# Moving the sum of tap products to TensorE, and reordering ScalarE and TensorE around the first turning, in a fused mix and two-FFN kernel

## The reference

```python
# per token s and head h: seven taps over the tokens s-6 .. s
w = softmax(weight_gen)                      # over the last axis, 7 taps
x = sum over k of w[s, h, k] * x_pad[s + k]  # 8 heads of 24 columns, D = 192
# gated FFN, 1536 wide
xn = x / sqrt(mean(x*x) + 1e-6) * rms_g
x = (silu(xn @ w_gate) * (xn @ w_val)) @ w_out
# second FFN, 2048 wide
h = x @ w_in
out = (h * (1 / (1 + exp(-1.702 * h)))) @ w_out2
```

## Time and profile before

| | us |
|---|---|
| median of 3 runs | 1227.09 |
| lowest, highest | 1226.65, 1227.09 |
| the profiled execution | 1227.05 |
| its span in the trace | 1225.1 |

### The profile page before, as it was taken

How to read it: one execution, slowest core, us unless ns; L and a number is a source line. 1 busy time by engine, 2 the same in 40 slices (tenths; PEclk the granted TensorE clock), 3 DMA queues, 4 the chain that set the end, 5 groups by cost and what they waited for, 6 DMA issues and landing times.

```text
span 1225.1 us, 28909 instructions
## 1 busy us (share of the span) xinstructions
PE 1214.6 (99%) x12025; PEld 1047.0 (85%) x12025; DVE 794.9 (65%) x1245; ACT 662.0 (54%) x1180; POOL 59.5 (5%) x65
## 2 busy tenths in 40 slices
PE   8999999999999999999999999999999999999998
PEld 5989999888898888988888888888988889888888
DVE  7887584855839567494774848658385674944533
ACT  5655555455554555646455454555645556454554
POOL 4323000000000000000000000000000000000000
PEclk9999999999999999999999999999999999999999
DMA  7220010100101001010010001000010010000000
GB/s 206 85 67 32 18 33 2 50 2 18 33 5 47 1 19 33 18 34 2 18 34 18 33 2 37 15 18 34 5 47 1 18 34 2 14 1 14 1 15 14
DMA packets 15457, 33.10 MB, mean 27 GB/s; under 512 B 1892, under 2 KB 8804, under 8 KB 15328
## 3 DMA queue, kind: packets, MB, share of 16 engines
q1 hardware_dynamic: 15328, 31.26, 8.0%
HBM read 24.96 MB, written 6.29 MB: 26 GB/s over the span
## 4 chain that ended last, share of the span: by engine, by line
PE 96%; DVE 1%; DMA 1%; ACT 1%; issue 0%; SPq 0%; POOL 0%; ACTq 0%; DVEq 0%
PE up_ps L996 52%; PE acc L996 40%; PE up_ps L1000 2%; PE acc L1000 2%; DMA x_win<-in_x_dram 0%; DMA stage<-in_moe_w_val_dram 0%; DVE h_lo L953 0%; PE acc L1260 0%; PE acc L1268 0%; DVE hidden L942 0%; ACT o_lo L610 0%; ACT h_hi L652 0%; ACT L628 0%; POOL rms_stat L502 0%; ACT hidden L645 0%
## 5 line engine op out<-in xcount | busy, mean ns | idle before, releaser
L953 DVE TENSOR_TENSOR h_lo<-hidden,h_hi 128x512 fp32r<-128x512 f32 x448 | 314.3, 702 | 320.9 <-ACT h_hi L652 320.4
L652 ACT CAST h_hi<-hidden 128x512 fp32r<-128x512 f32 x448 | 278.1, 621 | 244.9 <-DVE hidden L942 234.0
L996 PE MATMUL acc<-out_w,h_hi 64*128 64x384 f32 x1024 | 300.3, 354 | 0.0
L1000 PE MATMUL acc<-out_w,h_hi 64*128 64x384 f32 x1024 | 299.7, 353 | 0.0
L645 ACT ACTIVATE hidden<-up_ps 128x512 f32<-128x512 f32 x256 | 152.5, 596 | 193.8 <-PE up_ps L1000 193.6
L996 PE MATMUL acc<-out_w,h_lo 64*128 64x192 f32 x1024 | 253.1, 247 | 0.0
L1000 PE MATMUL acc<-out_w,h_lo 64*128 64x192 f32 x1024 | 253.0, 247 | 0.0
L996 PE MATMUL up_ps<-x_hi,up_w 64*128 64x512 f32 x752 | 236.7, 394 | 0.0
L1000 PE MATMUL up_ps<-x_hi,up_w 64*128 64x512 f32 x752 | 234.8, 392 | 0.0
L996 PE MATMUL acc<-h_hi,out_w 64*128 64x512 f32 x576 | 195.5, 393 | 2.4 <-DVE y_f L889 1.3
L996 PEld LDWEIGHTS acc<-out_w,h_lo 64*128 64x128 f32 x1024 | 191.3, 187 | 5.2
(11 more groups left out here) (145 smaller groups left out, 3202.8 us busy)
## 6 DMA issues: line engine op xcount, KB each, us to landing
x_win<-in_x_dram SPq DMA_DIRECT2D x14, 960.0 KB
out_dram<-out_sb SPq DMA_DIRECT2D x15, 384.0 KB, 2.3
stage<-in_moe_w_out_dram SPq DMA_DIRECT2D x13, 192.0 KB, 3.5
logits<-in_weight_gen_dram SPq DMA_DIRECT2D x16, 112.0 KB, 2.0
stage<-in_moe_w_in_dram SPq DMA_DIRECT2D x4, 256.0 KB, 2.9
stage<-in_moe_w_gate_dram SPq DMA_DIRECT2D x3, 256.0 KB, 5.0
stage<-in_moe_w_gate_dram SPq DMA_DIRECT2D x5, 128.0 KB, 4.9
stage<-in_moe_w_val_dram SPq DMA_DIRECT2D x5, 128.0 KB, 5.1
```

What stands on the lines that cost most here:

```text
L652: nc.scalar.copy(h_hi[:, u % 4, :], hidden[:, u % 2, :]).then_inc(hi_ready, 1)
L953: nc.vector.tensor_tensor(h_lo[:, u % 4, :], hidden[:, u % 2, :], h_hi[:, u % 4, :].bitcast(F32), ALU.subtract).then_inc(lo_ready, 1)
L996: return nc.tensor.matmul(ps, w[TOP], data[TOP], start=start, stop=stop)
L1000: return nc.tensor.matmul(ps, w[LOW], data[LOW], start=start, stop=stop)
```

## The change

TAPS_PE goes from 4 to 6: the first six products go to buffers of their own and TensorE adds them (two matmuls for each product, each recorded as two instructions); the seventh goes to `mixed`, and VectorE's two additions of products among themselves are gone. On ScalarE the squares of x(0) stand behind the first rounded copy and ahead of the second and third; copy_left(1) goes from ahead of copy 4 to behind round_main(0); the small Silu that loads its table, and copy 4, go behind copy_twin(0). Copies 6 and 7 go from ahead of block 0 into it (HI_FIRST 8 to 6). On TensorE leave(0) is followed by eight rehearsals, then leave(1), the turning and leave(2); the other rehearsals behind the taps are gone.

```diff
-    TAPS_PE = 4
+    TAPS_PE = TAPS - 1
...
-    HI_FIRST = 8
+    HI_FIRST = HI_POOL + 1
...
+        first_taps += [tap[:, 0, :, :], tap[:, 1, :, :]]
...
             mix_exp(0)
-            for n in range(3):
-                chunk_hi_half(n)
+            chunk_hi_half(0)
+            mix_square(0)
+            chunk_hi_half(1)
+            chunk_hi_half(2)
             copy_left(0)
-            mix_square(0)
             chunk_hi_half(3)
-            copy_left(1)
-            chunk_hi_half(4)
             mix_exp(1)
             act.wait_ge(g_ready, 2)
             round_main(0)
-            nc.scalar.activation(warm[:, :], g_main[:, :], ACT.Silu)
+            copy_left(1)
             copy_left(2)
             copy_twin(0)
-            for n in range(HI_POOL + 1, HI_FIRST):
-                chunk_hi_half(n)
+            nc.scalar.activation(warm[:, :], g_main[:, :], ACT.Silu)
+            chunk_hi_half(4)
             all_blocks(run)
...
-                    to = first_taps[k] if k < TAPS_PE else (mixed, tap[:, 0, :, :], tap[:, 1, :, :])[k - TAPS_PE]
+                    to = first_taps[k] if k < TAPS_PE else mixed
...
-                for k in range(TAPS_PE + 1, TAPS):
-                    dve.wait_ge(tapped, TAPS + k - TAPS_PE - 1)
-                    nc.vector.tensor_tensor(mixed, mixed, tap[:, k - TAPS_PE - 1, :, :], ALU.add).then_inc(tapped, 1)
-                dve.wait_ge(tapped, TAPS + TAPS - TAPS_PE - 1)
+                dve.wait_ge(tapped, TAPS)
...
             leave(0)
+            rehearse(up_ps[3], 8)
             leave(1)
-            rehearse(up_ps[3], 3)
+            turn_x(0)
             leave(2)
-            turn_x(0)
-            rehearse(up_ps[3], 3)
```

## The result

The kernel before took 1226.83 us (median of 13 runs side by side), the changed kernel 1229.67 us (1229.55 to 1229.91, 13 runs): 2.84 us more, a ratio of 1.0022 with a 95% interval of 1.0014 to 1.0029. The prediction said 1228.1, in a range up to 1229.4, and gave 88% to a change within 0.2%. The time lies outside the range and 0.4 us beyond that bound. The profiled executions took 1227.05 and 1229.67 us, spans 1225.1 and 1227.7, so the traces have 2.6 of the 2.84 us. The 13 times of the kernel before spread over 1.0 us (1226.63 to 1227.65), those of the changed kernel over 0.4: before, ScalarE's rounded copies stand ahead of the squares and wait for their chunks' loads, and in the six traces here with that order and four taps on TensorE the turning starts anywhere from 17.68 to 18.82; in the four with the changed kernel's order and six taps it starts at 18.89 to 19.04.

What follows compares the result with a forecast made beforehand. TensorE, busy 99% of the span, was taken as the bound. Block 0's 0.65 + 0.75 - 0.32 gave +1.1 us, part 3's 0.52 lying within it; 1227.05 + 1.1 made 1228.1 us, range 1226.6 to 1229.4.

Steps and rivals of the forecast that it cites:

- Parts 1 and 2: Before the first matmul: two more TensorE taps, +0.89 us; squares first gives about half back, leaving +0.45 us.
- Part 3: TensorE's order before the first matmul: turning at 18.75, first matmul at 20.4, stream then +0.52 us late.
- Part 4, silu(1): Block 0: silu(1), behind more rounded copies, makes VectorE's next product 0.65 us late, between 0.5 and 0.95.
- Part 4, the overlap: Block 0: GpSimd's later work overlaps VectorE's for 2 us more and stretches it; 0.75 us, between nothing and 3.3.
- slack of 0.32 us: Block 0: spare time between h_lo(5)'s end on VectorE and TensorE's use of it, taken off the sum.
- (b): Block 0: TensorE's 1.01 us stall at 27.88 absorbs the delay; +0.2 us (-0.2 to +0.3), 1227.25 us; 20%.
- (c): Block 0: h_lo(0) and followers run unstretched, stall closes; -0.5 us, 1226.55; 6%, and 2% for gains over 2.45 us.
- (d): Block 0: port contention makes both tap-product halves and h_lo(5) wait 1.10 us each; +3.9 us, 1231.0; 10% with smaller forms.

Runs made afterwards that it cites:

- b_hold5: Kernel before with one wait added: GpSimd's work on chunk 5 waits for h_lo(0), other engines' programs untouched; 1228.28 us against 1226.74.
- a_silu1: Changed kernel with ScalarE's copies 8 and 9 moved behind silu(1), most later copies about a unit later too; 1228.76 us against 1229.67.
- the three fixes: Changed kernel with four taps on TensorE, copy 4 ahead of round_main(0), and copies 8 and 9 behind silu(1); together 1227.10 us against 1226.74 before.
- b_hold8: Kernel before with GpSimd's split of chunk 8 waiting for h_lo(0); 1226.68 us against 1226.74.

## Why the prediction was wrong, step by step

**Parts 1 and 2, right.** The new taps stand 1.29 us apart (10.64, 11.93), the additions start at 14.78 (said: 14.65), the first square at 15.43 (15.27). VectorE sits idle for 2.96 us ahead of them: the 1.95 us of additions taken off it were time it did not need.

**Part 3, right in mechanism, some 0.25 us or more short.** The turning is at 18.96 (said: 18.75), leave(2) holds TensorE to the first matmul at 20.76 (20.4), and at the first matmul of the lower half of the array the stream is 22.48 - 21.71 = 0.77 us late (0.52). The two runs without GpSimd's reads give 1.1 us for the whole of the later x(0); the trace of before has a turning of 18.19, and other traces with its order start theirs up to 0.5 us earlier.

**Part 4, silu(1): right.** silu(1) starts at 27.76 (said: 27.5 to 27.9), the product behind it at 28.38, 0.73 us late (said: 0.65).

**Part 4, the overlap: the term that failed.** I took 0.75 us for it. VectorE's h_lo(5) ends at 46.04 + 0.68 = 46.72, 2.91 late; less the 0.73 of silu(1), the overlap cost 2.18 us. Row by row, 1.92 of that are three instructions at the end: the product of 192 columns at 40.02 took 1.10 us more than in the kernel before, h_lo(4) 0.55 and the addition at 43.10 0.27. Those lie beside the idle that GpSimd filled and its later end, the very overlap that I had priced. So the place was right, and length and price were not. Reckoned as in the forecast, the added overlap is the 0.75 us of idle and GpSimd's end, 4.03 us later, less VectorE's own 0.98 (40.02 for 39.04): 3.8 us and not 2, at 0.51 us lost for each and not 0.37. Two things were left out. First, I moved GpSimd by 3.0 us and it moved by 4.4 at chunk 5, and 4.0 at its end: the split of chunk 4 started at 24.24 and not 23.7, and took 1.81 us and not 1.14, and the cast took 1.09 and not 0.64, since they too now lie beside VectorE. Second, I left the stretches in between as they were, and they were dealt again. h_lo(0) lost 1 us less, but VectorE then waited for silu(1) anyway; behind that, the first product lost 0.27 more, h_lo(1) 0.52 and h_lo(2) 0.28 more, h_lo(3) 0.83 less. All that comes to only 0.25 us in sum. The slack of 0.32 us held: 0.73 + 2.18 - 0.32 = 2.59, and TensorE was 2.54 late at that point and 2.6 in the span.

**The rivals.** (b) and (c) counted on h_lo(0) being free, and it was, and the wait at 27.88 went: -0.6 us at that point against before. Neither came, for the reason given against (c), silu(1), and the splits that fell on h_lo(1). (d), the slower rival, is what came, in a smaller form: it wanted 1.8 of its 3.3 us to be real, and 2.18 were. Its mechanism was right and its instructions were not: both halves of the tap product (45.10 and 45.57) and h_lo(5) ran unstretched, at 0.55, 0.55 and 0.68 us, and three instructions ahead of them were hit. It got 10%, because I argued that GpSimd would be done by 43.1; it ended at 44.9.

**The rule.** The Trainium skill ("SBUF — State Buffer", Who interferes with whom) says that a VectorE instruction with two SBUF inputs contends with a GpSimd one that reads SBUF, not with one that only writes. The runs agree: 0.68 to 0.69 us in every h_lo beside a GpSimd that only writes, up to 1.78 beside one that reads. The rows also fit (d)'s reading, that each of two such instructions waits for the other's end. In the changed kernel the split at 29.96 ends at 31.82 and h_lo(1) at 32.37, the split at 41.33 ends at 42.63 and h_lo(4) at 43.18: both 0.55 us behind it, little less than h_lo's own 0.68. I put the collisions beside the sum; they belonged into it.

**What stays open.** Of GpSimd's share, 1.7 us, the runs don't say how much is stretched VectorE work and how much TensorE waiting for a split itself: in the changed kernel both waits end with an h_lo, in b_hold5 and a_silu1 two and one end with a split. The share of silu(1), 0.91 us in one run and none without GpSimd's reads, overlaps with that 1.7 and is not a third part. And the three fixes account for 2.57 of 2.84 us; the rest is within what these runs can tell.

## What to carry to other kernels

When two engines contend, moving one of them deals every collision behind the move again, and the moved engine is itself slowed, so it moves further than by its own delay. Go through the instructions that the added overlap can reach one by one. Where a follower's slack is only tenths of a microsecond, take the highest stretch that the trace shows, for two instructions, as the likely price and not as the rival: here 2 x 1.10 = 2.2 us against 2.18 measured, though one case does not make that a rule. And taking work off an engine gains nothing where the other half of the same sum ends later: ask first which side of a join is last.

## What the runs showed of the hardware

GpSimd and VectorE slow each other: with VectorE reading two operands from SBUF, h_lo took mostly 0.68, 0.95, 1.23 or 1.78 us, and GpSimd's split of 128x512 took 1.3 to 2.1 us. A GpSimd instruction that only writes left every h_lo at 0.68 to 0.69. The product with one operand in PSUM stayed at 0.67 to 0.69 us in block 0 of every trace. And removing one of these collisions was worth nothing in b_hold8 (1226.68 against 1226.74), though the instruction it freed became 1.1 us shorter.
